# Turning a head's row maxima in front of the product with V of the same tile

## The chip, the cores and the metric

The kernel runs on one core of one Trainium2 chip. The metric is the device time of one execution in microseconds (us), lower is better. Engines are named as in the profile: PE (TensorE matmuls), PEld (TensorE weight loads), DVE (VectorE), ACT (ScalarE), POOL (GpSimd), SP (SyncE, which only issues DMAs here).

## The reference, cut to what matters

```python
scores = scale * np.matmul(q, k.transpose(0, 1, 3, 2))     # 4 x 8 heads, 576 x 576 each
thresh = np.max(scores, axis=-1, keepdims=True) - tau
scores = np.where(scores >= thresh, scores, -1000000000.0)
scores = scores - np.max(scores, axis=-1, keepdims=True)
attn = np.exp(scores)
attn = attn / (np.sum(attn, axis=-1, keepdims=True) + 1e-09)
out = np.matmul(attn, v)                                   # 576 x 64 for each head
```

Each query row keeps only the keys whose score lies within tau of the row's maximum. The result goes through a layer of 8 experts (top 2 of 8, 512 to 1024 to 512) and a dense layer (512 to 2048 to 512). The change touches the attention alone, which takes the first 365 us.

## The kernel before, in words

**Tiles and slots.** There are 32 heads, and each head has 5 tiles: four of 128 rows and one of 64 (`NT = 5`). All engines walk through the same list of slots, `n = 5h + j`, one slot for a tile, written out in full without a loop on the chip; `i` and `c` in the code are `n // 20` and `n % 20`. Each engine has a function `slot` with its own share of a slot, and engines meet only through semaphores. PE carries out its instructions in the order in which they are written.

**What PE does in slot n.** Four things can stand in a slot, in this order before the change:

1. Scores S of tile n + 8 (L530, L531, 4 matmuls): query rows as output rows. DVE takes the row maxima from them (L976).
2. Transposed scores ST of tile n (L543, L544, 4 matmuls), with the negative row maxima added through extra rows of `q_lo`. ACT takes the exponential (L789) into `probs`, and DVE sets to zero what is below the threshold (L992, called the masking pass here). ACT and POOL then split `probs` into a high part (L797) and a low part (L1311).
3. The product with V of tile n - 3 (L560, 6 matmuls, 4 for the small tile), added up over a head's five tiles in `o_acc`, which is one buffer.
4. Only where j = 3: the turns. The row maxima of head h + 1 are turned from columns into rows (L570 x4, L571; called the turn of the maxima), and the finished output of head h - 1 is transposed (L577 x5, from `o_t`, a copy of `o_acc`).

With LAG = 3, the product with V in slot j = 3 is that of tile 0 of head h. It overwrites `o_acc`, so it waits until ACT has copied the output of head h - 1 to `o_t` (L826, semaphore `ot_out`). ACT makes this copy in slot j = 2, behind the exponential of that slot. The product also waits for POOL's low part (`lo_done`).

**Who waits for the turn of the maxima.** ACT copies the turned rows to `q_lo` (L838, behind `max_turned`) at the end of its slot j = 3, and DVE copies the small tile's part (L1018), which waits also for the transposes (`o_turned`). PE needs both two slots later, for ST of the next head. The values turned come from DVE (L984 to L997, semaphore `max_split`), made in slot j = 1.

**The ring.** S, ST and the turns write to `ring`, three places of two PSUM banks each, taken in turn. Each use has a number, in the order S, ST, turns within a slot; a use needs the place of the use three numbers before it. DVE counts `freed` up once for each use that it has read, in the same order. The turns and the transposes share one use, called "om".

```python
        for n in range(FIRST, LAST):
            f = max_rows_in(n // SL, n % SL)
            for kind, m, total in (("s", n + AHEAD, TILES), ("st", n, TILES),
                                   ("om", -1 if f is None else n // SL * U + f, NH + 2)):
                if 0 <= m < total:
                    numbers[kind][m] = sum(len(v) for v in numbers.values())

        def place_free(eng, kind, i, c):
            wait(eng, freed, use(kind, i, c) - 2)
```

**The other queues.** DVE in a slot: maxima of tile n + 8, masking pass of tile n, and where j = 3 the copy L1018 and the division that writes the output rows (L1029 to L1033). ACT in slot j = 1 also splits the queries and keys of head h + 3 (L805); POOL follows with their low part (L1316), and SP moves the parts between partitions by DMA (L432, L434, L439, L440). PE waits for the last of these DMAs in slot j = 2, before S of the first tile of that head. In eight of the slots from 22 on, 17 apart, ACT and POOL also split a piece of the first expert's weights (L835, L1321).

Of the kernel before, what the change touches and what calls it, by code (L numbers as in the profile page):

```python
# [6 lines left out]
P = 128  # L7
# [9 lines left out]
def build(nc, qk, v, tau, w_gate, w_noise, noise, w1, w2, w_in, w_out, alpha, out):  # L17
    B, H = qk.shape[:2]
    S, D = out.shape[0] // B, qk.shape[2] // 2
    NH = B * H  # L20
    NT = (S + P - 1) // P
    FULL = NT - 1
    TAIL = S - FULL * P
    SP = NT * P
    HALF = S // 2
    U = 4
# [29 lines left out]
    with ExitStack() as ctx, ExitStack() as attention_only:  # L56
# [32 lines left out]
        max_cols = sb("max_cols", [P, NT, D + 4], F32R)  # L89
        ident_r = sb("ident_r", [P, P], F32R)  # L90
# [10 lines left out]
        ring = ps("ring", [P, 3, 2, 512])  # L101
# [10 lines left out]
        max_turned = sem("max_turned"); max_in = sem("max_in"); max_tail_in = sem("max_tail_in")  # L112
# [22 lines left out]
        while sum(len(g) for g in groups) < TOK:  # L135
            at = sum(len(g) for g in groups)
# [30 lines left out]
        start = rb("start", [P, TOK, E])  # L167
# [118 lines left out]
        def tile(i, c):  # L286
            return i * SL + c

        def head(i, c):
            return i * U + c  # L290

        def has(i, c, total, per):

            return 0 <= i * per + c < total

        def wait(eng, s, count):
            if not isinstance(count, int) or count > 0:
                eng.wait_ge(s, count)
# [4 lines left out]
        MAX_TAIL = 384  # L303
# [13 lines left out]
        def copied(g):  # L317

            return (g - g % 2) // 2 * 32
# [26 lines left out]
        def max_rows_in(i, c):  # L346

            return c // NT + 1 if c % NT == 3 else None

        numbers = {"s": {}, "st": {}, "om": {}}  # L350
        for n in range(FIRST, LAST):
            f = max_rows_in(n // SL, n % SL)
# [4 lines left out]
        def use(kind, i, c):  # L357

            return numbers[kind][i * (SL if kind in ("s", "st") else U) + c]
# [5 lines left out]
        def place(kind, i, c):  # L365

            return use(kind, i, c) % 3

        def place_free(eng, kind, i, c):

            wait(eng, freed, use(kind, i, c) - 2)
# [136 lines left out]
        def _(pe):  # L508
# [4 lines left out]
            def slot(i, c):  # L513
                j = c % NT
                if has(i, c + AHEAD, TILES, SL):
                    m = c + AHEAD
                    t, g = m % NT, m // NT
                    s = g % U
                    cols = slice(t * P, t * P + P)
                    place_free(pe, "s", i, m)  # L520
                    if t == 0 and head(i, g) < BY_ENGINES:
                        wait(pe, highs_moved, head(i, g) * 2 + 2)
                        wait(pe, lows_moved, head(i, g) + 1)
                        wait(pe, own_rows_moved, head(i, g) + 1)
                    elif t == 0:
                        wait(pe, copies_in[s % 2], copied(head(i, g)))
                    for a in range(2):
                        half = slice(a * HALF, a * HALF + HALF)
                        dst = ring[:, place("s", i, m), a, 0:HALF]
                        pe.matmul(dst, q_hi2[:, s, cols], k_parts[:, s, half], start=True, stop=False)  # L530
                        mm = pe.matmul(dst, q_lo[0:D + 2, s, cols], k_ones[0:D + 2, s, half], start=False, stop=True)  # L531
                    mm.then_inc(s_ready, 1)
                if has(i, c, TILES, SL):
                    s = c // NT % U
                    cols = slice(j * P, j * P + P)
                    place_free(pe, "st", i, c)
                    if j == 0:
                        wait(pe, max_in, head(i, c // NT) + 1)
                        wait(pe, max_tail_in, head(i, c // NT) + 1)
                    for a in range(2):  # L540
                        half = slice(a * HALF, a * HALF + HALF)
                        dst = ring[:, place("st", i, c), a, 0:HALF]
                        pe.matmul(dst, k_parts[:, s, cols], q_hi2[:, s, half], start=True, stop=False)  # L543
                        mm = pe.matmul(dst, k_ones[0:D + 4, s, cols], q_lo[0:D + 4, s, half], start=False, stop=True)  # L544
                    mm.then_inc(st_ready, 1)
                if has(i, c - LAG, TILES, SL):
                    m = c - LAG
                    t, h = m % NT, m // NT
                    wait(pe, lo_done, tile(i, m) + 1)
                    if t == 0:  # L550
                        wait(pe, v_split, head(i, h) + 1)
                        wait(pe, ot_out, head(i, h))
                    if t == FULL:
                        wait(pe, v_tail_done, head(i, h) + 1)
                    products = ((v_hi, probs_hi), (v_lo, probs_hi), (v_hi, probs_lo)) if t < FULL else ((v_lo, probs_hi), (v_lo, probs_lo))
                    for a in range(2):
                        half = slice(a * HALF, a * HALF + HALF)
                        o = o_acc[0:D + 1, a, 0:HALF]
                        for n, (values, weights) in enumerate(products):
                            mm = pe.matmul(o, values[:, h % 2, t, 0:D + 1], weights[:, m % 4, half], start=(t == 0 and n == 0),  # L560
                                           stop=(t == FULL and n == 1))
                    mm.then_inc(pv_done, 1)
                f = max_rows_in(i, c)
                if f is not None and has(i, f, NH + 2, U):
                    place_free(pe, "om", i, f)
                if f is not None and has(i, f, NH, U):
                    at = ring[:, place("om", i, f)]
                    wait(pe, max_split, head(i, f) + 1)
                    for t in range(FULL):
                        mm = pe.matmul(at[0:D + 4, 1, t * P:t * P + P], max_cols[:, t, :], ident_r[:, :], start=True, stop=True)  # L570
                    mm = pe.matmul(at[0:D + 4, 0, MAX_TAIL:MAX_TAIL + TAIL], max_cols[:, FULL, :], ident_r[:, 0:TAIL], start=True, stop=True)  # L571
                    mm.then_inc(max_turned, 1)
                if f is not None and has(i, f - 2, NH, U):
                    h = f - 2
                    wait(pe, ot_out, head(i, h) + 1)
                    for t in range(NT):
                        mm = pe.transpose(ring[:, place("om", i, f), 0, t * (D + 2):t * (D + 2) + D + 1],  # L577
                                          o_t[0:D + 1, h % 2, t * P:t * P + P], ident[0:D + 1, 0:D + 1])
                    mm.then_inc(o_turned, 1)
            slots(pe, slot)  # L580


# [49 lines left out]
            for d in range(1, FIRST_TILES):  # L632
                mm = pe.matmul(first_ps[:, d:FIRST_TILES], ones_bf[:, :], mask_bf[:, 0:FIRST_TILES - d, 0],
                               start=False, stop=(d == FIRST_TILES - 1))
# [5 lines left out]
            for q in range(FIRST_TILES):  # L640
                if q in (0, FIRST_TILES // 2):
                    pe.wait_ge(first_at_ready, 1 if q == 0 else 2)
                mm = pe.matmul(sums_first, at_partition[:, q, :], tokens_first[:, q, :, :].rearrange("p k c -> p (k c)"),
                               start=(q == 0), stop=(q == FIRST_TILES - 1))
# [5 lines left out]
            for d in range(1, TOK):  # L650
                mm = pe.matmul(counts_ps[:, d * E:TOK * E], ones_bf[:, :], flat_mask[:, 0:(TOK - d) * E],
                               start=False, stop=(d == TOK - 1))
# [778 lines left out]
```

## Time and profile before

| what | value |
|---|---|
| time, median of 3 runs | 1315.56 us (1313.82 to 1316.27) |
| the profiled execution: its time, its span | 1315.53 us, 1313.8 us |
| busy over the span | PE 95%, PEld 86%, DVE 47%, POOL 43%, ACT 41% |
| attention | about 0 to 365 us; from there routing, experts, dense layer |
| mean granted TensorE clock | 0.986 |

The span is the time from the first to the last instruction of the one execution that the profiler recorded. Busy shares are means over stages with different limits, so for this change only the attention counts. Start times in rows are microseconds from the start of the span. Where a row has square brackets, they hold the idle time of the engine before the instruction and what ended it. PEld rows show best when PE really starts something, since the ends of the matmuls are modelled.

### The profile page before, as it was taken

Reading aid. Unit: us, or ns where it says so; the run is one execution under the profiler, and the core shown is the slowest. Engines: PE = TensorE matmul, PEld = TensorE weight load, DVE = VectorE, ACT = ScalarE, POOL = GpSimd, SP = SyncE. Lnnn points to the kernel's source line nnn. Section 1 sums busy time; section 2 is a strip of 40 time slices with the busy share of each in tenths; the row PEclk is TensorE's granted clock in tenths of the full one; section 3 lists DMA queues with packets and bytes.
Section 4 is the critical chain, followed back from the end, with each engine's and each line's share of the span. In section 5 each row is a group of like instructions: output and inputs, shape, how many; then the busy total and the mean of one; then the engine's idle time right before and its main releaser. Section 6 shows DMA issues by size and latency. Waiting matters only on the chain.

```text
span 1313.8 us, 20231 instructions
## 1 busy us (share of the span) xinstructions
PE 1244.9 (95%) x7678; PEld 1135.9 (86%) x7678; DVE 622.8 (47%) x1249; ACT 539.4 (41%) x966; POOL 568.8 (43%) x412
## 2 busy tenths in 40 slices
PE   5999999999885999999999999998999999999998
PEld 4899999989864889989999999997999999999997
DVE  7888888888745521212212121215544535444433
ACT  5777787878742243333333333333212112112111
POOL 5989999989810344343524434454511101000000
PEclk9999999999986999999999999999999999999999
DMA  5545454453520143343424333344221102000000
GB/s 174 129 120 139 125 148 125 128 135 100 168 52 25 57 153 111 130 129 96 132 93 144 101 123 125 105 161 128 82 73 49 32 1 73 16 0 24 16 1 25
DMA packets 71170, 123.14 MB, mean 94 GB/s; under 512 B 11824, under 2 KB 30512, under 8 KB 71088
## 3 DMA queue, kind: packets, MB, share of 16 engines
q1 hardware_dynamic: 57216, 86.90, 23.4%
q0 software_dynamic: 6080, 19.93, 4.9%
q10 hardware_dynamic: 7792, 15.21, 3.1%
q8 instruction: 52, 0.85, 0.3%
q14 instruction: 30, 0.25, 0.1%
HBM read 82.43 MB, written 19.92 MB: 78 GB/s over the span
## 4 chain that ended last, share of the span: by engine, by line
PE 79%; POOL 6%; issue 5%; ACT 4%; DVE 3%; DMA 2%; SPq 0%; ACTq 0%; POOLq 0%
PE h_ps L702 32%; PE y_ps L721 11%; PE y_ps L720 11%; PE y_ps L719 11%; PE o_acc L560 5%; POOL probs_lo L1311 4%; PE ring L530 2%; PE ring L531 2%; PE t_ps L680 2%; PE ring L544 2%; PE ring L543 2%; POOL k_parts L1316 1%; DMA k_parts<-k_ones 1%; ACT q_hi L805 1%; ACT probs_hi L797 1%
## 5 line engine op out<-in xcount | busy, mean ns | idle before, releaser
L702 PE MATMUL h_ps<-x_hi,region_a 128*128 128x384 f32 (+1 forms) x1408 | 343.8, 317 | 4.8 <-DVE x_lo L1203 4.3
L702 PEld LDWEIGHTS h_ps<-x_hi,region_a 128*128 128x128 f32 x1408 | 246.5, 189 | 11.6 <-DVE x_lo L1203 5.2
L1311 POOL TENSOR_TENSOR probs_lo<-probs,probs_hi 128x576 fp32r<-128x576 f32 x160 | 226.6, 1427 | 34.0 <-ACT probs_hi L797 34.0
L702 PE MATMUL h_ps<-x_lo,region_a 128*128 128x384 f32 (+1 forms) x704 | 221.2, 314 | 0.0
L1213 DVE SCALAR_TENSOR_TENSOR h_lo<-h_ps,h_hi 128x256 fp32r<-128x256 f32 (+1 forms) x128 | 62.8, 491 | 311.6 <-ACT h_hi L896 288.4
L899 ACT ACTIVATE h_hi<-act_out 128x384 fp32r<-128x384 f32 (+1 forms) x112 | 53.7, 480 | 312.3 <-DVE act_out L1224 305.8
L719 PE MATMUL y_ps<-region_b,h_hi 128*128 128x512 f32 x448 | 175.7, 392 | 1.4 <-DVE h_lo L1230 1.4
L720 PE MATMUL y_ps<-region_b,h_hi 128*128 128x512 f32 x448 | 176.5, 394 | 0.0
L721 PE MATMUL y_ps<-region_b,h_lo 128*128 128x512 f32 x448 | 176.5, 394 | 0.0
L1297 POOL TENSOR_TENSOR region_b<-stage,region_b 128x1024 fp32r<-128x1024 f32 x40 | 95.8, 2399 | 143.5 <-ACT region_b L778 143.4
L896 ACT ACTIVATE h_hi<-h_ps 128x256 fp32r<-128x256 f32 (+1 forms) x128 | 56.0, 437 | 240.2 <-PE h_ps L702 231.9
L1221 DVE TENSOR_SCALAR act_neg<-h_ps,alpha_sb 128x384 f32<-128x384 f32 (+1 forms) x112 | 62.8, 560 | 186.5 <-PE h_ps L702 180.1
L992 DVE SCALAR_TENSOR_TENSOR probs<-ring,threshold,probs 128x576 f32<-128x576 f32 x160 | 130.5, 816 | 42.5 <-ACT probs L789 41.5
L702 PEld LDWEIGHTS h_ps<-x_lo,region_a 128*128 128x128 f32 x704 | 133.4, 190 | 5.7
L789 ACT ACTIVATE probs<-ring 128x576 f32<-128x576 f32 x160 | 103.6, 647 | 64.0 <-PE ring L544 63.4
L1297 POOL TENSOR_TENSOR region_a<-stage,region_a 128x1024 fp32r<-128x1024 f32 x32 | 76.7, 2399 | 120.1 <-ACT region_a L778 120.1
L976 DVE TENSOR_REDUCE neg_max<-ring 128x1 f32<-128x576 f32 (+1 forms) x160 | 119.6, 748 | 10.7 <-PE ring L531 10.5
L702 PE MATMUL h_ps<-x_hi,region_b 128*128 128x384 f32 (+1 forms) x512 | 123.2, 312 | 0.7 <-issue 0.7
L530 PE MATMUL ring<-k_parts,q_hi 128*128 128x288 f32 x320 | 96.7, 315 | 20.4 <-DVE k_ones L962 14.9
L797 ACT ACTIVATE probs_hi<-probs 128x576 fp32r<-128x576 f32 x160 | 108.1, 675 | 0.8 <-DVE probs L992 0.7
L721 PEld LDWEIGHTS y_ps<-region_b,h_lo 128*128 128x128 f32 x448 | 84.1, 188 | 18.5
L719 PEld LDWEIGHTS y_ps<-region_b,h_hi 128*128 128x128 f32 x448 | 84.3, 188 | 15.7 <-DVE h_lo L1230 2.9
(202 smaller groups left out, 2406.3 us busy)
## 6 DMA issues: line engine op xcount, KB each, us to landing
stage<-in_moe_w SPq DMA_DIRECT2D x56, 512.0 KB
qk_raw<-in_qk SPq DMA_DIRECT2D x32, 320.0 KB, 3.4
expert_rows<-rows_out ACTq DMA_DIRECT2D x8, 768.0 KB, 3.9
v_nat<-in_v SPq DMA_DIRECT2D x16, 320.0 KB, 3.6
k_ones<-q_hi SPq DMA_DIRECT2D x30, 160.0 KB, 2.6
q_lo<-k_parts SPq DMA_DIRECT2D x30, 160.0 KB, 2.4
q_hi<-q_hi SPq DMA_DIRECT2D x30, 160.0 KB, 2.4
k_parts<-k_ones SPq DMA_DIRECT2D x30, 160.0 KB, 2.9
```

The source lines that it names most:

```text
L530: pe.matmul(dst, q_hi2[:, s, cols], k_parts[:, s, half], start=True, stop=False)
L560: mm = pe.matmul(o, values[:, h % 2, t, 0:D + 1], weights[:, m % 4, half], start=(t == 0 and n == 0), stop=(t == FULL and n == 1))
L702: mm = pe.matmul(h_ps[:, c % 2, 0:width], wt, x[kind][:, cc, :], start=(n == 0), stop=(n == 3 * C - 1))
L719: pe.matmul(y, h_hi[:, c % 4, cols], region[:, 0, off:off + DM], start=(f == 0), stop=False)
L720: pe.matmul(y, h_hi[:, c % 4, cols], region[:, 1, off:off + DM], start=False, stop=False)
L721: mm = pe.matmul(y, h_lo[:, c % 4, cols], region[:, 0, off:off + DM], start=False, stop=(f == fs - 1))
L789: act.activation(probs[:, c % 4, :].rearrange("p (a n) -> p a n", a=2), ring[:, place("st", i, c), :, 0:HALF], ACT.Exp, scale=SCALE).then_ ...
L797: act.activation(probs_hi[:, m % 4, :], probs[:, m % 4, :], ACT.Copy).then_inc(hi_done, 1)
L976: dve.tensor_reduce(neg_max[0:r, g % 2, t, 0:1].bitcast(F32), ring[0:r, place("s", i, m), :, 0:HALF], AX.XY, ALU.max, negate=True).then_in ...
L992: dve.scalar_tensor_tensor(kept_probs, ring[:, place("st", i, c), :, 0:HALF], threshold[:, 0:1], kept_probs, ALU.is_ge, ALU.mult).then_inc ...
L1297: pool.tensor_tensor(region[:, 1, cols], stage[:, j % RING, :], region[:, 0, cols].bitcast(F32), ALU.subtract).then_inc(w_lo, 1)
L1311: pool.tensor_tensor(probs_lo[:, m % 4, :], probs[:, m % 4, :], probs_hi[:, m % 4, :].bitcast(F32), ALU.subtract).then_inc(lo_done, 1)
```

## The change

In PE's slot the wait for the om place (`place_free`), the wait for `max_split` and the five matmuls of the turn of the maxima are moved from behind the product with V to in front of it. The transposes of head h - 1's output stay behind the product. Nothing is added or taken away, and no other engine's code changes.

```diff
                     mm.then_inc(st_ready, 1)
+                f = max_rows_in(i, c)
+                if f is not None and has(i, f, NH + 2, U):
+                    place_free(pe, "om", i, f)
+                if f is not None and has(i, f, NH, U):
+                    at = ring[:, place("om", i, f)]
+                    wait(pe, max_split, head(i, f) + 1)
+                    for t in range(FULL):
+                        mm = pe.matmul(at[0:D + 4, 1, t * P:t * P + P], max_cols[:, t, :], ident_r[:, :], start=True, stop=True)
+                    mm = pe.matmul(at[0:D + 4, 0, MAX_TAIL:MAX_TAIL + TAIL], max_cols[:, FULL, :], ident_r[:, 0:TAIL], start=True, stop=True)
+                    mm.then_inc(max_turned, 1)
                 if has(i, c - LAG, TILES, SL):
...
                     mm.then_inc(pv_done, 1)
-                f = max_rows_in(i, c)
-                if f is not None and has(i, f, NH + 2, U):
-                    place_free(pe, "om", i, f)
-                if f is not None and has(i, f, NH, U):
-                    at = ring[:, place("om", i, f)]
-                    wait(pe, max_split, head(i, f) + 1)
-                    for t in range(FULL):
-                        mm = pe.matmul(at[0:D + 4, 1, t * P:t * P + P], max_cols[:, t, :], ident_r[:, :], start=True, stop=True)
-                    mm = pe.matmul(at[0:D + 4, 0, MAX_TAIL:MAX_TAIL + TAIL], max_cols[:, FULL, :], ident_r[:, 0:TAIL], start=True, stop=True)
-                    mm.then_inc(max_turned, 1)
                 if f is not None and has(i, f - 2, NH, U):
                     h = f - 2
                     wait(pe, ot_out, head(i, h) + 1)
```

## Rows read from the trace of the kernel before

**Rows 1.** Busy time by engine, 42 to 349 us; last columns clock, DMA share, GB/s
```profile
42.00:349.00 307.00, 291.87 (x2258) 280.42 (x2256) 253.53 (x521) 242.00 (x443) 278.42 (x213) 1.00 0.50 134
```

**Rows 2.** Timeline, all engines, slot 3 of head 20 (start, duration, engine, line)
```profile
240.47 0.63 ACT L789 ACTIVATE probs<-ring 128x576 f32<-128x576 f32 x1
...
241.00 0.64 ACT L826 ACTIVATE o_t<-o_acc 65x576 f32<-65x576 f32 x1
...
241.13 0.82 DVE L992 SCALAR_TENSOR_TENSOR probs<-ring,threshold,probs 128x576 f32<-128x576 f32 x1 [0.74 <-ACT probs L789]
...
241.31 0.19 PEld L544 LDWEIGHTS ring<-q_lo,k_ones 68*128 68x128 f32 x1
...
241.75 0.13 PEld L560 LDWEIGHTS o_acc<-probs_hi,v_hi 128*65 128x65 f32 x1 [0.25 <-issue]
...
242.46 0.40 PEld L570 LDWEIGHTS ring<-ident_r,max_cols 128*68 128x68 f32 x4
...
242.87 0.39 PEld L577 LDWEIGHTS ring<-ident,o_t 65*128 65x128 f32 x5
...
243.07 0.59 ACT L838 ACTIVATE q_lo<-ring 4x512 fp32r<-4x512 f32 x1
```

**Rows 3.** Timeline, the same place in head 2
```profile
50.51 0.64 ACT L826 ACTIVATE o_t<-o_acc 65x576 f32<-65x576 f32 x1
...
50.65 0.82 DVE L992 SCALAR_TENSOR_TENSOR probs<-ring,threshold,probs 128x576 f32<-128x576 f32 x1 [0.78 <-ACT probs L789]
...
51.27 0.13 PEld L560 LDWEIGHTS o_acc<-probs_hi,v_hi 128*65 128x65 f32 x1 [0.29 <-issue]
```

**Rows 4.** Timeline, the same place in head 30
```profile
347.09 0.63 ACT L826 ACTIVATE o_t<-o_acc 65x576 f32<-65x576 f32 x1
347.22 0.82 DVE L992 SCALAR_TENSOR_TENSOR probs<-ring,threshold,probs 128x576 f32<-128x576 f32 x1 [1.22 <-ACT probs L789]
...
347.83 0.13 PEld L560 LDWEIGHTS o_acc<-probs_hi,v_hi 128*65 128x65 f32 x1 [0.79 <-POOL probs_lo L1311]
```

**Rows 5.** Timeline, the same place in head 8
```profile
114.36 0.82 DVE L992 SCALAR_TENSOR_TENSOR probs<-ring,threshold,probs 128x576 f32<-128x576 f32 x1 [0.81 <-ACT probs L789]
...
114.81 0.65 ACT L826 ACTIVATE o_t<-o_acc 65x576 f32<-65x576 f32 x1 [0.49 <-PE o_acc L560]
```

**Rows 6.** Timeline: PE released by a masking pass, in head 3
```profile
58.50 0.82 DVE L992 SCALAR_TENSOR_TENSOR probs<-ring,threshold,probs 128x576 f32<-128x576 f32 x1
...
59.42 0.19 PEld L530 LDWEIGHTS ring<-k_parts,q_hi 128*128 128x128 f32 x1 [1.14 <-DVE probs L992]
```

**Rows 7.** The chain of waits: first turn of the maxima in it from head 1 on, two neighbours, and the last
```profile
41.85 0.25 PE ring L570 x4
...
232.46 0.25 PE ring L570 x4
...
242.75 0.25 PE ring L570 x4
...
348.84 0.25 PE ring L570 x4
```

**Rows 8.** The chain of waits where it passes by the turn of head 14
```profile
175.55 0.73 ACT q_hi L805
...
182.85 3.80 DMA k_parts<-k_ones
```

**Rows 9.** Timeline of weight loads: idle time of PE behind the turns of heads 5, 14, 22
```profile
90.95 0.19 PEld L530 LDWEIGHTS ring<-k_parts,q_hi 128*128 128x128 f32 x1 [0.43 <-issue]
...
186.75 0.19 PEld L530 LDWEIGHTS ring<-k_parts,q_hi 128*128 128x128 f32 x1 [0.69 <-issue]
...
271.68 0.19 PEld L530 LDWEIGHTS ring<-k_parts,q_hi 128*128 128x128 f32 x1 [1.55 <-DVE probs L992]
```

**Rows 10.** Timeline of weight loads, slot 3 of heads 9 and 28
```profile
126.06 0.13 PEld L560 LDWEIGHTS o_acc<-probs_hi,v_hi 128*65 128x65 f32 x1 [0.56 <-POOL probs_lo L1311]
...
327.21 0.13 PEld L560 LDWEIGHTS o_acc<-probs_hi,v_hi 128*65 128x65 f32 x1 [1.08 <-POOL probs_lo L1311]
```

## The prediction

> **What bounds the kernel now.** I read four views, in this order. First the busy times by stretch: the change touches only the attention, and of the 307 us between head 1's and head 30's turns PE is busy for 291.87 and POOL for 278.42 [rows 1]. So PE is nearly full and POOL close behind it. Then the chain of waits over the attention, asking only whether it goes through the turn of the maxima in each head: it does in 20 of the 30 heads from 1 to 30; the first and the last are in [rows 7]. In the other ten it goes from ACT over POOL, or over POOL and two DMAs, straight to a later matmul of PE [rows 8]. Then the timeline of one ordinary head, to see what PE waits for in slot 3 [rows 2]. Last, the same few instructions in every other head, by the timeline of the weight loads and of DVE and ACT [rows 3 to 5, 10].
>
> In the ordinary head, the exponential of slot 2 releases two things at once: ACT's copy of the output (L826, 241.00 + 0.64 = 241.64) and DVE's masking pass (L992, 241.13 + 0.82 = 241.95). PE issued its last ST load until 241.50, then stands, and starts the product with V at 241.75, 0.11 behind the copy [rows 2]. Head 2 shows the same (51.15, PE at 51.27) and so does head 30 (347.72, PE at 347.83) [rows 3, 4]. Going through all 30 heads, the product starts 0.11 us behind the end of the copy in 29; only in head 18 does POOL's low part come later. An idle time that the profile puts down to POOL there is in truth one for the copy [rows 4]. From the product on PE runs without a gap: product 0.71 us (241.75 to 242.46), turn 0.41 (242.46 to 242.87), transposes, next slot [rows 2]. Two neighbouring heads with nothing else in the way are 242.75 - 232.46 = 10.29 us apart [rows 7].
>
> **What is moved.** Five matmuls, 0.41 us of PE by the weight loads [rows 2], the same five as before; no DMA and nothing of SP's or POOL's queue. Taken as work alone the move costs 0. What it also moves is the wait for the place in the ring, and this decides. The om use has number u; in its slot ST has u - 1 and S has u - 2. The wait wants `freed` at u - 2, so everything up to number u - 3 read, and that is ST of the slot before, j = 2. It is DVE's masking pass of slot 2 that frees it. The second wait, `max_split`, is met since slot 1 and costs 0.
>
> **When the place comes free.** The masking pass ends at 241.95 [rows 2]. The nearest row for the way from the end of a masking pass to a waiting PE gives 59.42 - (58.50 + 0.82) = 0.10 us [rows 6]. So the turn can start at 242.05. Before, it came at 242.46, and the wait for the place was hidden under the 0.71 us of the product; now nothing covers it. Queued behind the waiting turn on PE are the product of tile 0, the transposes, and S and ST of slot 4, for which DVE and ACT wait.
>
> The new order in this head: turn 242.05 to 242.46, product to 242.46 + 0.71 = 243.17, then the transposes, which started at 242.87 before. The stretch ends 0.30 us later. The formula is (end of masking pass + 0.10) - (end of copy + 0.11), because turn plus product are the same 1.12 us in either order. In head 2 it gives (51.47 + 0.10) - 51.27 = 0.30, in head 30 (348.04 + 0.10) - 347.83 = 0.31 [rows 3, 4]. It is this steady because both are released by the same exponential, and a masking pass takes 0.82 us where a copy takes 0.64 and starts 0.13 earlier. PE's own idle time does not enter: where it stood 0.56 us for the copy it will stand 0.86 [rows 10].
>
> **Which heads.** The order of the two ends is the other way round where ACT's copy had itself to wait for PE: in head 8 the masking pass ends at 115.18 and the copy at 115.46 [rows 5], so turn and product end at the old time, cost 0. Heads 1 and 25 are like it. Head 18 has POOL's wait, and no loss. That leaves 26 heads with about 0.30 each.
>
> **What of it lies on the path.** Of the 20 turns in the chain, those of heads 1, 8 and 25 cost 0, which leaves 17. Each of these lies on a stretch of the chain in which the exponential of slot 2 leads to PE's product and from there to the next head, so the lengthened stretch is 17 x 0.30 = 5.1 us. The other nine delayed heads are passed by: in head 14 the chain runs from ACT (175.55) over POOL and DMAs [rows 8] to PE at 186.75, where PE had stood for 0.69 us [rows 9]. I looked for such an idle time behind each of the nine, before the chain comes back to PE, and found from 0.43 to 1.55 us, always more than 0.30 [rows 9]. They take the delay in, cost 0. If that cover were missing, it would be 9 x 0.30 = 2.7 us more, 7.8 in all, which is the upper bound.
>
> **What comes earlier.** The turned maxima are ready 0.41 us earlier than before. ACT's copy (L838) starts at 243.07, right behind the turn, with ACT's split of probs before it ending at about 243.0, so it gains 0.07 us at most [rows 2]; PE needs these rows only two slots later. Then ACT stands for ST of slot 4, which now comes 0.30 us later. DVE's copy (L1018) waits for the transposes too, which come later. So nothing is gained: 0. The product of tile 0 ends 0.71 us later than before where 0.30 is lost (243.17 against 242.46), but `pv_done` of it is wanted by ACT only two slots on, and nobody is late for it: 0. SP's store of output rows waits for DVE's division, 0.3 us later, in a queue with slack: 0.
>
> **The sum.** 1315.53 us (the profiled execution, its span of 1313.8 included) + 5.1 = 1320.6 us. The median of the runs shown is 1315.56, so the reference point is the same within 0.03.
>
> **A rule against this change.** The rows show PE standing at a load while later work is queued, for example 1.14 us before an S tile [rows 6]; they do not by themselves show that a ready product behind it could not have gone ahead. The Trainium skill, "TensorE: Matmul & The Clock Gate", section "Step-by-step: what each phase is for", says that weight loads may be pulled ahead of running matmuls but that the matmuls themselves keep program order. By that rule a turn that waits holds the product; without it the product could pass and the sum would be near 0. The trace fits the rule, as every row above can be read in program order.
>
> **The rivals.**
>
> *The gap is filled (faster).* PE stood before the product in most heads, 0.25 to 0.56 us [rows 2, 10]. If the place were free by then, the turn would lie in that gap and each head would win the gap, at most 0.41. Over the 17 heads of the chain the gaps, each cut at 0.41, add up to 4.5 us: 1311.0 us. It decides where the masking pass ends before PE's last ST load, at 241.50 in [rows 2] instead of 241.95. For it speaks that such an order exists [rows 5]; against it, that there PE had no gap, and that 26 of 30 heads have the masking pass 0.3 us behind the copy. Chance 0.07.
>
> *The delay does not reach the end (no change).* POOL has 278.42 us of work in 307 [rows 1]; if its queue or the DMAs really set the pace in more heads than the chain tells, or a waiting turn does not hold the product, 5.1 shrinks below 2.6 us: 1315.5 to 1318. For it speaks that ten heads are passed by already [rows 8]; against it, that the ordinary heads are 10.29 us apart with no POOL in the chain. Chance 0.13.
>
> *More than counted.* All delayed heads add up, or ACT and DVE, now pushed 0.3 us, miss a further slot. Beyond the 7.8 us: 1324 to 1327. For it speaks nothing but the tightness of all engines. Chance 0.03. A lower clock is part of this: the granted clock stays at full speed, 2.4 GHz, through the attention [rows 1] with an idle time of 1.55 us in it [rows 9], while the longest wait that I expect for the turn is 1.08 + 0.31 = 1.39 us [rows 10], so I leave it out of the sum.
>
> **How the numbers follow.** The forecast, 17 to 26 heads at 0.30 us with some give for DMAs that fall otherwise, has the chance 0.77 and its own range 1318.3 to 1323.5. The range for 8 in 10 reaches down into the case of no change and ends a little above the upper bound: 1316.8 to 1323.8. A measurement of this kernel can tell about 0.2%, 2.6 us, from no change. Slower by more than that: 0.77 + 0.03 = 0.80; within it 0.13; faster 0.07.
>
> **What the profile after would show.** The loads of L570 stand in front of L560 in slot 3, with idle time before them that ends with DVE's masking pass (probs, L992) in some 26 heads, 0.3 us longer than the product's old idle time, some 17 us in all (the old gaps of these heads add up to 9.8, and 26 x 0.30 is 7.8). L560 of tile 0 follows without a gap. Ordinary neighbouring heads are 10.6 us apart instead of 10.29, heads passed by stay as far apart as they were, and the first transposes after the attention start some 5 us later than before; behind that all is as before. The prediction is wrong if the loads of L570 start right behind ST, or if neighbours stay at 10.3 us.

## The result, and the profile after

The change makes the kernel slower: 1318.59 us (median of 20 runs, 1316.78 to 1321.29) against 1315.70 us for the kernel before (20 runs, 1313.57 to 1318.07), ratio 1.0022 with a 95% interval of 1.0016 to 1.0028, so 2.9 us more. A second comparison gave 1.0027 (1.0017 to 1.0037), 3.5 us more. The forecast was 5.1 us more.

First the waits of the changed kernel, 42 to 352 us (who waited for whom, us in total, times, longest):

```profile
PEld ring L553 <- DVE probs L992: 18.3, 26, 1.3
...
DVE q_lo L1018 <- PE ring L577: 9.0, 26, 0.4
```

The loads of the turn (now L553) wait 26 times, 18.3 us in all, for DVE's masking pass. The prediction named 26 heads and some 17 us. That the counts agree is partly luck, for they are not the same 26: head 30, which I had counted, does not wait (below), and head 18, which I had left out because POOL's low part held its product, does, for 0.82 us. The second row shows that DVE's copy of the turned rows, which needs the transposes too, comes no earlier: the same row of the kernel before is 3.2 us in 15 waits.

Now one ordinary head, number 10, in the timeline; its rows answer to [rows 2]:

```profile
136.01 0.19 PEld L544 LDWEIGHTS ring<-q_lo,k_ones 68*128 68x128 f32 x1
136.03 0.63 ACT L826 ACTIVATE o_t<-o_acc 65x576 f32<-65x576 f32 x1
136.16 0.82 DVE L992 SCALAR_TENSOR_TENSOR probs<-ring,threshold,probs 128x576 f32<-128x576 f32 x1 [0.90 <-ACT probs L789]
...
137.03 0.32 PEld L553 LDWEIGHTS ring<-ident_r,max_cols 128*68 128x68 f32 x4 [0.82 <-DVE probs L992]
...
137.33 0.14 PEld L570 LDWEIGHTS o_acc<-probs_hi,v_hi 128*65 128x65 f32 x1
...
138.06 0.47 PEld L577 LDWEIGHTS ring<-ident,o_t 65*128 65x128 f32 x5
...
138.44 0.20 PEld L530 LDWEIGHTS ring<-k_parts,q_hi 128*128 128x128 f32 x1
```

The copy is done at 136.66 and the product could start 0.11 later. It stands behind the turn, which waits for the masking pass (136.98) and starts at 137.03, so the product starts at 137.33. That is the rule on program order which the prediction took from the Trainium skill ("TensorE: Matmul & The Clock Gate", "Step-by-step: what each phase is for"), and the trace agrees: POOL's low part for this product was done by 136.37, so the turn alone stood in front, and the product's load came 0.67 us behind the copy instead of 0.11.

The load rows also give the size of the loss, piece by piece, against head 20 of before [rows 2], from one load start to the next. The first load of slot 4 behind head 20 of before is this one:

```profile
243.17 0.20 PEld L530 LDWEIGHTS ring<-k_parts,q_hi 128*128 128x128 f32 x1
```

| piece | before | after |
|---|---|---|
| end that releases PE, relative to the end of the copy | 0 | +0.32 (masking pass) |
| from there to PE's first load | 0.11 | 0.05 |
| turn | 0.41 | 0.30 |
| product | 0.71 | 0.73 |
| transposes, to the first load of slot 4 | 0.30 | 0.38 |
| sum | 1.53 | 1.78 |

So 0.25 us is lost in such a head, where I had said 0.30. Ordinary neighbours are indeed 10.53 us apart by the starts of their transposes (L577), 10.29 before.

Head 30 is the exception that I had missed:

```profile
350.28 0.40 PEld L553 LDWEIGHTS ring<-ident_r,max_cols 128*68 128x68 f32 x4
350.38 0.63 ACT L826 ACTIVATE o_t<-o_acc 65x576 f32<-65x576 f32 x1
...
350.52 0.82 DVE L992 SCALAR_TENSOR_TENSOR probs<-ring,threshold,probs 128x576 f32<-128x576 f32 x1 [1.22 <-ACT probs L789]
...
351.13 0.13 PEld L570 LDWEIGHTS o_acc<-probs_hi,v_hi 128*65 128x65 f32 x1 [0.39 <-POOL probs_lo L1311]
```

Here the turn starts at 350.28, long before the masking pass ends (351.34), and lies in PE's idle time; what was 0.79 us of it [rows 4] is 0.39. In the last slots no S tile is left, a slot uses one place of the ring fewer, and the place of the turn is then the one that the masking pass of the slot before last has freed. It is the gap-filling rival, in one head, and that head wins: the transposes of heads 29 and 30 are 9.64 us apart instead of 9.96.

### The profile page after: what moved, and what is told of

Read it like the earlier page. It is cut to its first block, busy times and chain, and to the rows that moved or that the text cites. A ratio compares the mean times of both kernels' runs of the same rounds, so it can differ in the third digit from the quotient of the medians.

```text
span 1315.8 us, 20231 instructions
## 1 busy us (share of the span) xinstructions
PE 1243.1 (94%) x7678; PEld 1135.0 (86%) x7678; DVE 622.1 (47%) x1249; ACT 538.8 (41%) x966; POOL 568.6 (43%) x412
## 4 chain that ended last, share of the span: by engine, by line
PE 78%; POOL 6%; issue 5%; ACT 4%; DVE 4%; DMA 2%; SPq 0%; ACTq 0%; POOLq 0%
PE h_ps L702 32%; PE y_ps L721 11%; PE y_ps L720 11%; PE y_ps L719 11%; PE o_acc L570 4%; POOL probs_lo L1311 3%; PE ring L530 2%; PE t_ps L680 2%; PE ring L531 2%; PE ring L544 2%; PE ring L543 2%; ACT probs_hi L797 1%; ACT q_hi L805 1%; POOL k_parts L1316 1%; DMA k_parts<-k_ones 1%
## 5 line engine op out<-in xcount | busy, mean ns | idle before, releaser
L1311 POOL TENSOR_TENSOR probs_lo<-probs,probs_hi 128x576 fp32r<-128x576 f32 x160 | 226.7, 1427 | 37.2 <-ACT probs_hi L797 37.0
```

What stands on the lines that cost most here:

```text
L1311: pool.tensor_tensor(probs_lo[:, m % 4, :], probs[:, m % 4, :], probs_hi[:, m % 4, :].bitcast(F32), ALU.subtract).then_inc(lo_done, 1)
```

## The experiments

Each kernel ran in five rounds against the kernel before. The two last columns are worked out from the traces: the usual distance of ordinary neighbouring heads (the median over heads 10, 13, 17, 21, 24, 27, starts of the transposes), and the stretch from head 1's first transpose to the first transpose behind the attention (L594 of the two kernels compared). The stretch leaves out what comes before, where the traces differ by up to 4 us. The first turn of the maxima starts anywhere from 21.5 to 23.0 us, without regard to the kernel. From there to the stretch it is 20.3 to 20.4 us in eleven traces, but 21.1 in the late masking pass with the new order, and 23.2 and 22.9 in the two kernels that share the key parts; there the change itself costs time, which comes back below.

| kernel | ratio to before (95%) | heads apart, us | stretch, us |
|---|---|---|---|
| before | 1 | 10.29 | 324.1 |
| changed | 1.0022 (1.0016 to 1.0028) | 10.53 | 327.6 |
| changed, again | 1.0027 (1.0017 to 1.0037) | 10.53 | 327.6 |
| the wait alone in front | 1.0041 (1.0027 to 1.0056) | 10.55 | 327.9 |
| short masking pass, old order | 1.0007 (0.9998 to 1.0015) | 10.30 | 324.2 |
| short masking pass, new order | 0.9990 (0.9979 to 1.0001) | 10.27 | 323.4 |
| the same and short POOL, old order | 0.9978 (0.9968 to 0.9987) | 10.29 | 321.4 |
| the same and short POOL, new order | 0.9950 (0.9938 to 0.9962) | 10.09 | 317.7 |
| turn between the product's halves | 1.0005 (0.9996 to 1.0014) | 10.29 | 324.4 |
| copy in two halves, old order | 0.9985 (0.9976 to 0.9995) | 10.28 | 324.0 |
| late masking pass, old order | 0.9997 (0.9988 to 1.0006) | 10.30 | 324.5 |
| late masking pass, new order | 1.0029 (1.0018 to 1.0041) | 10.62 | 329.0 |
| key parts shared with DVE | 0.9968 (0.9958 to 0.9978) | 10.30 | 319.0 |
| both: key parts shared, copy in halves | 0.9944 (0.9931 to 0.9958) | 10.05 | 316.0 |

**The changed kernel again.**

> The changed kernel once more, for a second trace and a second interval. Theory M (the turn waits for the masking pass of slot 2, which ends 0.25 us too late for PE in the heads on the path): 1.0020 to 1.0030 of the kernel before, and in the trace about 26 turns whose wait ends with a masking pass. If the idle stretch behind the attention was also shorter because of the change, the stretch from the first transposes behind the attention to the end is 1 us shorter again; if that was scatter, it lies anywhere within 1 us of the 947.7 us of before.

The attention takes the same 327.6 us and the waits are the same. From the first transposes behind the attention to the end, before had 1313.8 - 366.1 = 947.7 us, and this trace 1315.3 - 369.8 = 945.5. The kernel with the short masking pass in the old order has 944.2. So that stretch scatters by some 3 us whatever the order is, and the spans of single traces are no measure of a 3 us change; the stretch of the attention and the medians are.

Of the 3.4 us that the stretch grew in these two traces, 0.28 us is not the turn but TensorE's clock. These rows cover the last transposes of the attention, in the kernel before and in the changed one (stretch; busy time and count of PE, PEld, DVE, ACT, POOL; clock, DMA share, GB/s):

```profile
364.50:365.30 0.80, 0.50 (x5) 0.39 (x5) 0.17 (x1) 0.00 (x0) 0.00 (x0) 1.00 0.00 0
...
367.50:368.30 0.80, 0.75 (x5) 0.62 (x5) 0.00 (x0) 0.00 (x0) 0.00 (x0) 0.50 0.00 0
```

The granted clock falls from 2.4 to 1.2 GHz at the end of the attention in both. In the kernel before it falls between 365.0 and 365.5, behind the last transposes (364.55), in the changed kernel between 367.0 and 367.5, just before them (367.51), and the way from there to L594 takes 1.82 us instead of 1.54. The idle times of PE before are nearly the same (1.35, 0.65 and 1.08 us in the changed kernel, 1.37, 0.65 and 1.09 in the kernel before). The clock falls before the last transposes in both traces of the changed kernel and in the new order with the two short passes, but not with the wait alone, so no run ties it to the change.

**The wait alone.** The five matmuls stay behind the product; only `place_free` moves.

```diff
+                f = max_rows_in(i, c)
+                if f is not None and has(i, f, NH + 2, U):
+                    place_free(pe, "om", i, f)
                 if has(i, c - LAG, TILES, SL):
...
                     mm.then_inc(pv_done, 1)
-                f = max_rows_in(i, c)
-                if f is not None and has(i, f, NH + 2, U):
-                    place_free(pe, "om", i, f)
                 if f is not None and has(i, f, NH, U):
```

> Old order of the matmuls, but the wait for the om place stands in front of the product with V. M: the wait alone carries the loss, so the same 1.0020 to 1.0030 as the whole change, 2.6 to 4 us. Rival O (the loss comes from the order of the matmuls themselves, for example that turn and product follow each other badly on PE): 1.0000, no loss.

The loss is there in full, 1.0041. That is above the 1.0020 to 1.0030 that I expected, but its interval overlaps those of the change, and the stretch is 327.9 against 327.6. The weight loads of PE in head 10 of this kernel (product L563, transposes L577):

```profile
138.99 0.13 PEld L563 LDWEIGHTS o_acc<-probs_hi,v_hi 128*65 128x65 f32 x1 [0.82 <-DVE probs L992]
...
140.10 0.39 PEld L577 LDWEIGHTS ring<-ident,o_t 65*128 65x128 f32 x5
```

The product itself now waits 0.82 us for the masking pass. The order of the matmuls is not what costs; the wait is.

**A short masking pass, in both orders.** The masking pass of each head's third tile covers 144 of the 576 columns and leaves out the rest; it ends 0.13 us before the copy instead of 0.32 behind it.

```diff
+                    scores = ring[:, place("st", i, c), :, 0:HALF]
+                    if j == 2:
+                        kept_probs, scores = kept_probs[:, 0, 0:144], scores[:, 0, 0:144]
-                    dve.scalar_tensor_tensor(kept_probs, ring[:, place("st", i, c), :, 0:HALF], threshold[:, 0:1], kept_probs,
+                    dve.scalar_tensor_tensor(kept_probs, scores, threshold[:, 0:1], kept_probs,
```

> Old order; DVE's masking pass of slot 2 of each head covers only 144 of the 576 columns (the rest of the masking of that tile is left out), so it takes about 0.3 us instead of 0.82 and ends before ACT's copy. It is the reference for its partner in the new order. M: in the old order the pass is waited for by nothing on the path, so 0.9990 to 1.0005. If DVE as a whole is near the path, up to 0.997.

> New order with the same short masking pass (the same part left out). M: the place is free before PE's last ST load in most heads, so the turn fills the idle time in front of the product: 3 to 4.5 us less than the same kernel in the old order, 0.9965 to 0.9980 of it. Rival O (order of the matmuls costs by itself): 2 to 3 us more than its partner. Rival N (the gap in front of the product is not worth anything, because POOL or DMAs set the pace): equal to its partner.

In the old order the pass makes no difference. In the new order the loss is gone, as it must be if the pass is its cause. But the gain that I expected is not there: 1313.08 us against 1314.33, 1.25 us, not 3 to 4.5, with intervals that overlap and stretches 0.8 us apart, and the heads are still 10.27 apart. The timeline of the new order, head 10 and the start of its next slot, shows what took it:

```profile
137.26 0.64 ACT L826 ACTIVATE o_t<-o_acc 65x576 f32<-65x576 f32 x1
...
137.58 1.56 POOL L1319 TENSOR_TENSOR k_parts<-qk_raw,q_hi 128x640 fp32r<-128x640 f32 x1
137.81 0.32 PEld L553 LDWEIGHTS ring<-ident_r,max_cols 128*68 128x68 f32 x4 [0.35 <-DVE probs L995]
...
138.84 0.46 PEld L577 LDWEIGHTS ring<-ident,o_t 65*128 65x128 f32 x5
139.11 2.81 POOL L1314 TENSOR_TENSOR probs_lo<-probs,probs_hi 128x576 fp32r<-128x576 f32 x2
...
140.58 0.13 PEld L570 LDWEIGHTS o_acc<-probs_hi,v_hi 128*65 128x65 f32 x1 [0.24 <-POOL probs_lo L1314]
```

The transposes start 0.94 us behind the end of the copy (137.90); in head 10 of the kernel before it is 1.24, so PE did win 0.30 in slot 3. Then it stands 0.24 us in slot 4 for POOL's low part of the second tile: that pass is the first of the two from 139.11 on, so it ends at 139.11 + 1.40 = 140.51, as POOL had made `k_parts` first. In the kernel before the same two ends fell together without a wait: POOL's pass ended at about 242.83 + 1.40 = 244.23 and PE's product started at 244.30, right behind its last ST load (244.29), in head 20:

```profile
241.31 1.56 POOL L1316 TENSOR_TENSOR k_parts<-qk_raw,q_hi 128x640 fp32r<-128x640 f32 x1
...
242.83 2.81 POOL L1311 TENSOR_TENSOR probs_lo<-probs,probs_hi 128x576 fp32r<-128x576 f32 x2
...
244.10 0.19 PEld L544 LDWEIGHTS ring<-q_lo,k_ones 68*128 68x128 f32 x1
...
244.30 0.13 PEld L560 LDWEIGHTS o_acc<-probs_hi,v_hi 128*65 128x65 f32 x1
```

So two chains of equal length cross an ordinary head. Whatever makes PE's longer costs in full; what makes it shorter is worth next to nothing. The pair of kernels that follows tests this.

**POOL out of the way, in both orders.** On top of the short masking pass, POOL makes the low part of each head's second tile for 288 of 576 columns only, from head 1 on; the rest of that part is left out.

```diff
+                    width = HALF if j == 2 and tile(i, m) >= NT else S
-                    pool.tensor_tensor(probs_lo[:, m % 4, :], probs[:, m % 4, :], probs_hi[:, m % 4, :].bitcast(F32),
-                                       ALU.subtract).then_inc(lo_done, 1)
+                    pool.tensor_tensor(probs_lo[:, m % 4, 0:width], probs[:, m % 4, 0:width],
+                                       probs_hi[:, m % 4, 0:width].bitcast(F32), ALU.subtract).then_inc(lo_done, 1)
```

> Old order, short masking pass in slot 2 as before, and in addition POOL makes the low part of each head's second tile for only 288 of its 576 columns (the other half of that low part is left out), so that POOL reaches the end of this low part some 0.7 us earlier. Reference for its partner. Theory P (in ordinary heads POOL's chain, k_parts and then the low part of the second tile, is just as long as PE's, so that it takes away any gain of PE in slot 3): the old order gains little by itself, 0 to 3 us from the heads that POOL sets, 0.9975 to 1.0005.

> New order with the same two shortenings (the same parts left out). P: with POOL out of the way the turn in the gap is worth something, 1.5 to 3.5 us less than its partner, and ordinary neighbouring heads come closer than 10.3 us. Rival Q (the gain is capped by something else, ACT or the DMAs of the key parts): within 1 us of its partner, heads still 10.3 us apart.

This settles it. Without POOL's tie the new order is worth 1311.65 - 1308.84 = 2.8 us, 3.7 us by the stretches, and ordinary heads are 10.09 apart where the old order, with the same short POOL pass, stays at 10.29. Two neighbouring heads of the new order, weight loads:

```profile
126.69 0.46 PEld L577 LDWEIGHTS ring<-ident,o_t 65*128 65x128 f32 x5
...
135.76 0.32 PEld L553 LDWEIGHTS ring<-ident_r,max_cols 128*68 128x68 f32 x4 [0.22 <-DVE probs L995]
...
136.79 0.46 PEld L577 LDWEIGHTS ring<-ident,o_t 65*128 65x128 f32 x5
```

The rival "gap filled" was right about the mechanism and needs both: a place that is free in time, and a POOL that is not level with PE.

**The turn between the product's halves.** Three matmuls of the product, then the wait and the turn, then the other three.

```diff
+                        if a == 0 and f is not None:
+                            turn_maxima()
                     mm.then_inc(pv_done, 1)
```

> The turn of the maxima, with its wait for the place, stands between the first three and the last three matmuls of the product with V of slot 3. M (only the wait for the masking pass costs): the product starts 0.11 us behind the copy as in the old order, its first half takes 0.36 us and the place is free 0.3 us behind the copy, so the wait is covered: 0.9995 to 1.0007 of the kernel before, no wait for a masking pass in front of the turn. Rival O (breaking the order of the matmuls costs): 1.001 or more.

1.0005, heads 10.29 apart. Head 10, weight loads (first half of the product L573, turn L555):

```profile
137.59 0.13 PEld L573 LDWEIGHTS o_acc<-probs_hi,v_hi 128*65 128x65 f32 x1 [0.56 <-POOL probs_lo L1318]
137.91 0.40 PEld L555 LDWEIGHTS ring<-ident_r,max_cols 128*68 128x68 f32 x4
```

The turn starts 0.32 us behind the product, with no idle time before it. Three matmuls are enough cover for the wait, and breaking the product up costs nothing that can be measured.

**The copy in two halves, old order.**

```diff
-                    act.activation(o_t[0:D + 1, h % 2, 0:S].rearrange("p (a n) -> p a n", a=2), o_acc[0:D + 1, :, 0:HALF],
-                                   ACT.Copy).then_inc(ot_out, 1)
+                    for a in range(2):
+                        act.activation(o_t[0:D + 1, h % 2, a * HALF:a * HALF + HALF], o_acc[0:D + 1, a, 0:HALF],
+                                       ACT.Copy).then_inc(ot_out, 1)
```

The first three matmuls of the product wait for the first half, the others for the second.

> Old order, but ACT copies the output in two halves of 288 columns and the first half of the product waits only for the first copy, so the product starts some 0.2 us earlier in the ordinary head. If the path through slot 3 were the only one: 0.2 us in some 15 heads, 3 us, 0.9977. Theory P: POOL's chain ends at the same time and takes it away: 0.9990 to 1.0005, heads still 10.3 us apart. Two copies cost ACT more than one, so a small loss is possible.

0.9985, a little better than the 0.9990 that the tie allows at most, but far from 0.2 us in each head: the six distances are between 10.07 and 10.68, a shorter one paid for by a longer one. The stretch is 324.0 us against 324.1, so the trace does not show where the small gain in the medians comes from; it stays open.

**A late masking pass, in both orders.** DVE fills a scratch tile behind the exponential of slot 2, before the pass.

```diff
+                    if j == 2:
+                        dve.memset(filler[:, :], 0.0)
```

> Old order; in slot 2 of each head DVE first fills a scratch tile of 200 columns, between the end of the exponential and the masking pass, so the pass ends later by the fill's length (some 0.2 to 0.3 us, the trace will tell). M: in the old order the place is wanted 0.45 us after it comes free, so the delay is covered: 0.9995 to 1.0010 of the kernel before, heads 10.3 us apart.

> New order with the same fill. M: each turn waits longer by the length of the fill, so ordinary heads are 10.53 us plus that length apart, and with 14 or more heads on the path the kernel is 3 to 5 us above the new order without the fill, 1.005 to 1.007 of the kernel before. Rival O (the new order costs a fixed amount that has nothing to do with the masking pass): as the new order without the fill, 1.002 to 1.003.

Head 10 in the new order, copy, fill, masking pass and turn:

```profile
138.63 0.63 ACT L827 ACTIVATE o_t<-o_acc 65x576 f32<-65x576 f32 x1
138.84 0.23 DVE L993 MEMSET filler<- 128x200 f32 x1 [0.97 <-ACT probs L790]
138.98 0.69 DVE L995 SCALAR_TENSOR_TENSOR probs<-ring,threshold,probs 128x576 f32<-128x576 f32 x1
139.73 0.32 PEld L554 LDWEIGHTS ring<-ident_r,max_cols 128*68 128x68 f32 x4 [0.92 <-DVE probs L995]
```

The fill takes 0.23 us but delays the end of the pass by only 0.09: the pass starts 0.14 behind the fill's start, so the two rows overlap, and takes 0.69 instead of 0.82. It ends 0.41 us behind the copy instead of 0.32. The new order answers with just these 0.09: heads 10.62 apart instead of 10.53. The stretch is 329.0 instead of 327.6, and up to the last transposes, which leaves out the 0.28 us of the clock, 327.5 instead of 325.7. So it grew by 1.7 us, where 14 to 16 times 0.09 is 1.3 to 1.4; the rest is within the scatter of single heads. The old order does not answer, 0.9997. My 3 to 5 us rested on the fill's own length and was too large, and in the ratio alone (1.0029 against 1.0022 and 1.0027) the 1.4 us do not stand out; the traces carry this one. The 0.7 us more in front of the stretch go with the clock again: the turn at 30.94 waits 0.91 us for its masking pass, and from 31.0 to 34.3 us the granted clock is at 1.2 GHz (0.52), where the changed kernel had 1.00.

**A version that is faster.** If POOL and PE tie, both must get shorter. DVE takes half of POOL's `k_parts`:

```diff
+                if g is not None and has(i, g, NH, U) and head(i, g) >= LO_FIRST:
+                    wait(dve, qk_hi_done, head(i, g) + 1)
+                    dve.tensor_tensor(k_parts[:, g % U, 0:SP // 2], qk_raw[:, g % U // 2, g % 2, 0:SP // 2],
+                                      q_hi2[:, g % U, 0:SP // 2].bitcast(F32), ALU.subtract).then_inc(qk_lo_half, 1)
...
-                    pool.tensor_tensor(k_parts[:, g % U, :], qk_raw[:, g % U // 2, g % 2, :],
-                                       q_hi2[:, g % U, :].bitcast(F32), ALU.subtract).then_inc(qk_lo_done, 1)
+                    pool.tensor_tensor(k_parts[:, g % U, SP // 2:SP], qk_raw[:, g % U // 2, g % 2, SP // 2:SP],
+                                       q_hi2[:, g % U, SP // 2:SP].bitcast(F32), ALU.subtract).then_inc(qk_lo_done, 1)
```

> Old order; DVE makes one half (320 columns) of the low part of keys and queries that POOL made alone, so POOL's chain in slot 1 is some 0.78 us shorter, with all work done. P (POOL sets the heads that are 10.8 us or more apart and ties with PE in the others): the ordinary heads stay at 10.3 us, the long ones lose up to 0.5 us each, 2 to 5 us in all, 0.996 to 0.9985. If DVE, which is put in the way of its own masking pass, is the tighter one: 1.000 or above.

> Old order, with the copy in two halves and the halved key parts together. P: with POOL shorter, the earlier product is worth its 0.2 us in the ordinary heads too, 10.1 us apart, so 2 to 4 us below the halved key parts alone, 0.993 to 0.997. If the sum is only that of the two alone (0.9985 times that of the key parts), the tie with POOL was not what held the copy in halves back.

Sharing alone gives 0.9968: ordinary heads stay at 10.30, and several of the long ones shrink (heads 11 to 12 from 11.00 to 10.34, heads 22 to 23 from 11.31 to 10.29). With the copy in halves added, the ordinary heads come down to 10.05, and the kernel to 1308.17 us, 0.9944 of before. The product of the two alone would be 0.9968 x 0.9985 = 0.9953, within the interval, so the ratio alone does not prove that they help each other; the distance of the heads does, since its median moved in neither of the two. The timeline around slot 3 of head 10 in the version with both:

```profile
136.26 0.87 POOL L1323 TENSOR_TENSOR k_parts<-qk_raw,q_hi 128x320 fp32r<-128x320 f32 x1
136.44 0.14 PEld L562 LDWEIGHTS o_acc<-probs_hi,v_hi 128*65 128x65 f32 x1 [0.25 <-POOL probs_lo L1318]
137.09 2.82 POOL L1318 TENSOR_TENSOR probs_lo<-probs,probs_hi 128x576 fp32r<-128x576 f32 x2
```

`k_parts` takes POOL 0.87 us instead of 1.56, and PE's idle time in front of the product is 0.25 instead of 0.56.

Both kernels lose part of this again before the stretch begins, 2.8 and 2.5 us, so the stretch flatters them: with shared key parts alone it is 5.1 us shorter than before, the median of the time 3.8. The place is in head 0, here in the kernel with shared key parts alone:

```profile
28.61 0.19 PEld L531 LDWEIGHTS ring<-k_parts,q_hi 128*128 128x128 f32 x1 [2.11 <-DVE neg_max L977]
28.80 1.67 DVE L1003 TENSOR_TENSOR k_parts<-qk_raw,q_hi 128x320 fp32r<-128x320 f32 x1
31.19 0.29 PEld L544 LDWEIGHTS ring<-q_hi,k_parts 128*128 128x128 f32 x1 [0.94 <-DVE neg_max L977]
```

PE waits 2.11 and 0.94 us for DVE, whose new half of `k_parts` takes 1.67 us here and 0.48 at 42.22. Then the granted clock is 0.50 (1.2 GHz) from 31.0 to 37.2 us, where the kernel before has 1.00 throughout. Leaving the sharing out in head 0 was not tried, nor was the new order on top of both: its masking pass would still end behind the copy.

## Why the prediction was right, and where it was off

**The mechanism.** The step "when the place comes free" holds in every head but 30: the turn waits for DVE's masking pass of slot 2 in 26 heads, the pass ends 0.32 us behind the copy, and the product stands behind the turn. Head 30 is the one place where the count of ring uses was not redone: with no S tiles left, another use frees the place. The step "which heads" was wrong on head 18 too: POOL's low part did not hold it in the changed kernel, and its turn waited like the others. The wait alone brings the loss, a short pass takes it away, a later one makes it larger, and a cover of three matmuls hides it. The side and the range were right too. But 2.9 us is little more than half of 5.1, and the rival "the delay does not reach the end" took in everything below 2.6.

**The size in one head.** The step "the new order in this head" took turn plus product as the same 1.12 us in either order and the release as 0.10 us. Measured, the release is 0.05, the turn behind idle time takes 0.30 instead of 0.41, the product 0.73 instead of 0.71, and the transposes behind it 0.38 instead of 0.30. The last three almost cancel (-0.01 us together), so the 0.05 us of the release is the error: the net is 0.25 us, not 0.30. The row for the release was misread: in [rows 6] PE started 0.10 us behind a masking pass, that of slot 1, by chance. S of slot 2 needs the place freed by the pass of slot 0, which ended long before, and the end of the DMA of the key parts. In the changed kernel the same S load starts before the pass of slot 1 ends:

```profile
58.62 0.82 DVE L992 SCALAR_TENSOR_TENSOR probs<-ring,threshold,probs 128x576 f32<-128x576 f32 x1
59.21 0.19 PEld L530 LDWEIGHTS ring<-k_parts,q_hi 128*128 128x128 f32 x1 [0.81 <-issue]
```

59.21 is before 59.44, so nothing waited for that pass. The chain of waits of the changed kernel goes to this S through the DMA:

```profile
47.96 0.73 ACT q_hi L805
...
55.90 3.21 DMA k_parts<-k_ones
```

**The number of heads.** The step "what of it lies on the path" counted 17. The stretch grew by 327.6 - 324.1 = 3.4 us, of which 0.28 is the clock at the last transposes; 3.15 is left. Head 30 gave 0.32 back, so the other heads lost 3.5 us together, and 3.5 / 0.245 = 14. Two of the missing three are known: head 2, whose turn was in the chain of before only because the profile took that DMA for a masking pass, and head 30. The third is not pinned to a head: the DMAs of the key parts land up to 0.3 us earlier or later from trace to trace, and heads 3, 7 and 23 moved by as much. The nine heads that are passed by took the delay in, as said, within this scatter.

**What comes earlier is worth nothing.** Right, as far as the traces show: in head 10 ACT's copy of the turned rows starts at 137.79, just when ACT is through with its split of `probs` (137.08 + 0.68), and DVE's copy waits for the transposes longer than before.

**The rivals.** "The gap is filled" stands or falls, I wrote, with the time at which the masking pass ends. That was half of it; with the pass made short, POOL's tie with PE kept the gain to 1.25 us, and only with both out of the way was it 2.8. "The delay does not reach the end" had the tie right as a fact (POOL has 278.42 us in 307 [rows 1]) and its consequence wrong: a tie caps gains, not losses. Nothing came of "more than counted" in the heads: from 42 to 349 us the granted clock stayed at full speed (2.4 GHz), and no idle time before a turn there was above 1.35 us. But the clock was not quite nothing, as I had put it: its fall before the last transposes is 0.28 us of the 3.4, and a turn that waited 0.91 us in head 0 of the late masking pass was followed by 3.3 us at 1.2 GHz.

## What to carry to other kernels

Before moving work in front of other work on an in-order engine, list every wait that moves with it and when each is met; here the five matmuls were free and the wait for a buffer, until then hidden under the product, was the whole price. Where two engines' chains have equal length, a shorter one gains nothing and a longer one costs in full, so test a small reorder with the other chain out of the way before calling the idea good or bad. A releaser that a profile names for a wait should be held against the code's count of what the semaphore needs, above all if a duration is to be taken from it. A stretch of the trace that leaves out scatter can leave out a cost as well: sharing the key parts loses 2.8 us in head 0 of the 5.1 that it wins behind it.

## What the runs showed of the hardware that was not expected

PE starts 0.05 us behind the end of the DVE pass that it waits for, and 0.11 us behind the end of the ACT copy. The same five small matmuls take 0.30 us from their first load to the next instruction's behind an idle time, and 0.38 to 0.41 us directly behind other matmuls. The stretch behind the attention takes 944 to 948 us without regard to the change under test; what sets it is open. The granted clock fell to 1.2 GHz within the attention in three kernels, in head 0, and each time PE had stood for a wait of 0.9 us or more shortly before (0.91 at 30.94 with the late masking pass, 2.11 and 0.94 at 28.61 and 31.19 with shared key parts). Longer waits than 0.91 us later in the attention (1.35 us in head 28 of the changed kernel) did not bring it down, so the length of one wait does not decide it.
